# The fifth tile of probabilities transposed with its 64 rows instead of 128

## The reference

```
k_p = k.reshape(B, H, 72, 8, D).mean(axis=3)          # keys and values pooled by 8
v_p = v.reshape(B, H, 72, 8, D).mean(axis=3)
scores = scale * q @ k_p^T                            # 576 x 72 for each head
attn = exp(scores - max) / (sum(exp) + 1e-9)
x = (attn @ v_p), heads side by side                  # 4608 x 512
x = (s * relu(x @ w_in)**2 + b) @ w_out               # 512 -> 2048 -> 512
x = silu(x @ w_in2) @ w_out2                          # 512 -> 2048 -> 512
```

## Time and profile before

| | |
|---|---|
| median of 3 runs | 1610.76 us (1609.34 to 1618.12) |
| the profiled execution | 1614.69 us, of which the span of the instructions is 1612.9 us |
| mean granted TensorE clock | 0.993 of full speed |
| transpositions (line 765) | 320, of which 64 are of a fifth tile |

### The profile page before, as it was taken

How to read it: one execution, slowest core, us unless ns; L and a number is a source line. 1 busy time by engine, 2 the same in 40 slices (tenths; PEclk the granted TensorE clock), 3 DMA queues, 4 the chain that set the end, 5 groups by cost and what they waited for, 6 DMA issues and landing times.

```text
span 1612.9 us, 23115 instructions
## 1 busy us (share of the span) xinstructions
PE 1576.1 (98%) x9220; PEld 1518.2 (94%) x9220; DVE 1034.5 (64%) x1087; ACT 879.2 (55%) x1024; POOL 236.8 (15%) x280
## 2 busy tenths in 40 slices
PE   7999989999999999999999999999999999999998
PEld 6999989998999999999999999999999999999998
DVE  5788788577665578467557846754674673475264
ACT  4675665754645654554575465547545545753442
POOL 4230130132220122112012211201111000000000
PEclk8999999999999999999999999999999999999999
DMA  5899898998998666777867667777766678666665
GB/s 162 307 363 362 330 349 346 360 323 284 310 338 299 230 232 231 241 242 272 262 229 237 236 229 241 276 264 238 233 226 232 209 274 271 222 223 224 223 226 180
DMA packets 120793, 424.88 MB, mean 263 GB/s; under 512 B 12912, under 2 KB 12912, under 8 KB 118640
## 3 DMA queue, kind: packets, MB, share of 16 engines
q1 hardware_dynamic: 117424, 413.98, 74.5%
q10 hardware_dynamic: 3264, 9.44, 1.5%
HBM read 346.95 MB, written 76.41 MB: 262 GB/s over the span
## 4 chain that ended last, share of the span: by engine, by line
PE 90%; DVE 4%; DMA 3%; ACT 2%; issue 1%; POOL 0%; SPq 0%; DVEq 0%; ACTq 0%; POOLq 0%
PE a_ps L908 21%; PE a_ps L885 20%; PE b_ps L908 15%; PE b_ps L885 15%; PE a_ps L811 3%; PE a_ps L835 3%; PE t_ps L746 2%; PE t_ps L765 2%; PE t_ps L778 2%; PE t_ps L835 2%; DMA xa_dram<-probs 1%; PE b_ps L811 1%; PE b_ps L835 1%; DMA ring<-w_dram 1%; PE a_ps L786 1%
## 5 line engine op out<-in xcount | busy, mean ns | idle before, releaser
L885 PE MATMUL a_ps<-xc_hi,ring 128*128 128x432 f32 (+1 forms) x1280 | 360.4, 348 | 2.8 <-DMA ring<-w_dram 1.2
L908 PE MATMUL a_ps<-sp_hi,ring 128*128 128x432 f32 (+1 forms) x1280 | 348.3, 347 | 2.3 <-DMA ring<-w_dram 2.3
L885 PE MATMUL b_ps<-xc_hi,ring 128*128 128x432 f32 (+1 forms) x960 | 273.7, 349 | 1.0 <-DVE gq L1350 1.0
L1389 DVE TENSOR_TENSOR sp_lo<-gq,sp_hi 128x1728 fp32r<-128x1728 f32 (+3 forms) x130 | 192.8, 1503 | 116.2 <-ACT sp_hi L1087 115.8
L908 PE MATMUL b_ps<-sp_hi,ring 128*128 128x432 f32 (+1 forms) x960 | 261.0, 346 | 0.0
L885 PEld LDWEIGHTS a_ps<-xc_hi,ring 128*128 128x128 f32 x1280 | 235.5, 189 | 12.0 <-ACT gq L1113 1.5
L908 PEld LDWEIGHTS a_ps<-sp_hi,ring 128*128 128x128 f32 x1280 | 235.4, 189 | 10.6 <-issue 2.8
L885 PE MATMUL a_ps<-xc_lo,ring 128*128 128x432 f32 (+1 forms) x640 | 222.0, 347 | 0.0
L908 PE MATMUL a_ps<-sp_lo,ring 128*128 128x432 f32 (+1 forms) x640 | 221.6, 346 | 0.0
L885 PEld LDWEIGHTS b_ps<-xc_hi,ring 128*128 128x128 f32 x960 | 176.5, 188 | 7.2 <-DVE gq L1350 1.4
L908 PEld LDWEIGHTS b_ps<-sp_hi,ring 128*128 128x128 f32 x960 | 175.9, 188 | 5.9
(11 more groups left out here) (169 smaller groups left out, 2456.0 us busy)
## 6 DMA issues: line engine op xcount, KB each, us to landing
ring<-w_dram SPq DMA_DIRECT2D x560, 512.0 KB, 4.2
w_dram<-w_stage SPq DMA_DIRECT2D x32, 1024.0 KB, 6.0
w_dram<-ring SPq DMA_DIRECT2D x48, 512.0 KB, 5.6
w_raw<-weights SPq DMA_DIRECT2D x16, 1024.0 KB, 7.0
k_stage<-kT SPq DMA_DIRECT2D x30, 288.0 KB, 4.5
q_sb<-qT SPq DMA_DIRECT2D x30, 288.0 KB, 4.7
v_stage<-vP SPq DMA_DIRECT2D x30, 288.0 KB
xa_dram<-probs SPq DMA_DIRECT2D x28, 288.0 KB, 4.7
```

The source lines that it names most:

```text
L885: last = nc.tensor.matmul(bank[:, half, 0:th], w, xc_of(x, th)[:, j, k, :], start=(first and k == 0 and i == 0), stop=(k == 1 and i == 2), ...
L908: last = nc.tensor.matmul(bank[:, m, 0:th], w, split_of(g, th, turn, 2 * c + half), start=(first and half == 0 and i == 0), stop=(end and ...
L1389: nc.vector.tensor_tensor(dst, src, hi, ALU.subtract).then_inc(dlo_ready, 1)
```

## The change

The fifth transposition of each group reads the 64 partitions of `probs` that hold real queries, multiplies them with the upper left 64 x 64 corner of the identity, and writes 64 columns of PSUM in place of 128. The other four stay as they are.

```
-                        g = 2 * j + e
-                        last = nc.tensor.transpose(flat(bank)[0:SP, j * P:(j + 1) * P], buf["probs"][:, g * SP:(g + 1) * SP],
-                                                   ident[:, :])
+                        g, rows = 2 * j + e, min(P, S - j * P)
+                        last = nc.tensor.transpose(flat(bank)[0:SP, j * P:j * P + rows],
+                                                   buf["probs"][0:rows, g * SP:(g + 1) * SP], ident[0:rows, 0:rows])
```

## The result

The changed kernel is slower: 1627.82 us against 1611.46 us, medians of six runs each, ratio 1.0097 with a 95% interval of 1.0077 to 1.0118. That is 15.6 us by the ratio (12.4 to 19.0). The forecast was 1610.3 us, no change that can be told; what happened is the first rival, the 64-row instruction that does not overlap with its neighbours, near the 1627 us that it named.

A forecast was written before the change was run, and what follows sets the result against it. TensorE was taken to bound the kernel; 0.1 us from 56 later groups and 0.4 us from the first 40 us gave 0.5 us off, so 1610.3 us from a median of 1610.76, range 1607.0 to 1633.0 us.

The forecast's parts named there:

- the first rival: At each fifth transposition, the 64-row instruction does not overlap with its neighbours: 5.4 to 26.2 us slower; chance 0.15 plus 0.33.
- What bounds the kernel: TensorE, busy 98% of the span; each change of its time counts in full from 57 us on.
- What one shorter transposition can give: A fifth transposition with 64 columns streams 0.055 us instead of 0.109, so at most 54 ns less at full clock.
- The stall moves from streaming to loading: Behind the fifth transposition in 56 later groups, a 128-column load hides the gain: 1 to 2 ns left each, 0.1 us.
- Going from 72 rows to 128 costs nothing: Matmuls of lines 778 and 811 start 0.13 to 0.14 us apart across the row change, so no cost was expected.
- a cheap and a dear part: Slower case for the 64-row transpositions, split by total cost: up to 8 us, chance 0.15; beyond 8 us, 0.33.
- The rival's price: Per fifth transposition without overlap: 0.193 us in place of 0.109, 84 ns more, plus the emptying time twice.
- The rival's own middle: Over all 64 groups, the middle of the slower case's costs above 8 us: some 16 us, giving 1627 us.
- The limit of 8 / 64: Added cost per group, put at 0.126 us, from which the slower case exceeds the 8 us a measurement can tell.
- The first 40 us: Eight early groups, some with short loads behind the fifth transposition, were to gain 0.38 us, at least nothing.

The follow-up runs named there:

- e1: The fifth transposition of each group takes 65 rows and 65 columns, against the kernel before the change: ratio 1.0001 (0.9978 to 1.0023).

## Why the prediction was wrong

- *What bounds the kernel*: right. TensorE's added time came out in full, 64 x 0.26 = 16.5 us against 15.6 measured (12.4 to 19.0).
- *What one shorter transposition can give*: right in size. The nine 64-row loads are 0.054 us apart, where 0.055 was read from the earlier trace rows.
- *The stall moves from streaming to loading*: right, and shown apart from the switch: with 65 rows nothing is gained in front of a 128-column load and 0.04 us in front of a 72-column one.
- *The step that failed* is "Going from 72 rows to 128 costs nothing", taken for 64 rows as well. The earlier trace rows hold for 72 rows, and e1 shows that they hold for 65; at 64 it is another case. What the runs show in its place is 0.26 us a group, 0.19 in front of the 64-row load and 0.07 behind it. The Trainium skill's page "TensorEngine Tiling (Array Packing)", Key Properties, says that changing the tiling mode drains TensorE. By that rule, the trace agrees: a hole at each change between 64 rows and more, and none among nine 64-row instructions. I gave this case 0.48 against 0.44 for the forecast, but split it into a cheap and a dear part and let the forecast stand as the likeliest.
- *The rival's price* had the right form. Nothing overlapped gave 0.084 us, and the emptying time came on top twice, with 0.05 and 0.163 us as the two values tried. An estimate from the trace: the four full streams of the group at 59.07 us end at 59.07 + 4 x 0.109 = 59.51, the fifth load starts at 59.59, 0.08 later. Behind it, 0.18 us less 0.03 of load and 0.055 of stream leave 0.10. So some 0.09 on each side, and 0.084 + 2 x 0.09 = 0.264 us. This shares out the measured 0.26 and is no second measurement of it; what supports it is that the price foreseen from it for another load behind (0.076 us less) and for a second pair of switches (0.30 us more) came out at 0.08 and 0.29. The rival's own middle, 16 us, is almost the 15.6 measured. That is luck in part: no row shown gave 0.09 us, and the middle was taken between two far bounds (5 and 26 us). (The limit of 8 / 64 is 0.125 us a group, not 0.126.)
- *The first 40 us*: no gain to be seen; the runs differ there by the clock (0.88 and 0.97 granted in the first 57 us).

What stays open: what the 0.09 us consist of. "Emptying" is a name for them; no run separates it from a restart of the reads. No run has fewer than 64 rows, or 64 rows in the upper half of the partitions.

## What to carry to other kernels

A matmul of 64 rows among matmuls of more is not a smaller matmul but two switches: here 0.26 us for one that saves 0.054 us of stream. Keep one row more than 64 (65 rows cost no switch) or gather the 64-row instructions, which run at full rate among themselves. And shorten a stream only where the load behind it is shorter still: put the short matmul in front of one with few columns of weights. The gain from that stands in the trace alone (0.04 us a group) and was too small for the runs.

## What the runs showed of the hardware

- The border lies between 64 and 65 rows: 1.0097 against 1.0001. That it is the rows and not the columns is shown by the plain matmuls, 1.0167 for 64 rows by 128 columns and 1.0013 for 128 by 64.
- A switch costs more at half clock. In the changed kernel's group at 394 us (granted clock 0.50 from 394.3 to 396.0 us) the hole before the fifth load is 0.38 us, not 0.19, while a step of 128 columns takes 0.215 us and not 0.109. The load behind comes 0.25 us after the fifth, not 0.18:

```profile
394.34 0.62 PEld L765 LDWEIGHTS t_ps<-ident,probs 128*72 128x72 f32 x4 [3.61 <-DVE probs L1266]
...
395.34 0.13 PEld L765 LDWEIGHTS t_ps<-ident,probs 64*72 64x72 f32 x1 [0.38 <-issue]
395.59 0.29 PEld L885 LDWEIGHTS a_ps<-xc_hi,ring 128*128 128x128 f32 x1
```

- A plain float32 matmul takes two loads and two matmuls, so line 746's 290 in the earlier trace rows are 145 tiles; a float32 transposition takes one of each, and its 72-column load is done in 0.03 us where a 128-column one takes 0.11.
